# First two heads in pieces, over two queues, in an attention and gated-layer kernel

## The reference, cut to what matters

```python
# 4 batches x 8 heads, 576 positions, head size 64, all float32
scores = scale * np.matmul(q, k.transpose(0, 1, 3, 2))
thresh = np.max(scores, axis=-1, keepdims=True) - tau
scores = np.where(scores >= thresh, scores, -1000000000.0)
scores = scores - np.max(scores, axis=-1, keepdims=True)
attn = np.exp(scores)
attn = attn / (np.sum(attn, axis=-1, keepdims=True) + 1e-09)
x = np.matmul(attn, v)                     # 4 x 576 x 512 after the heads are joined
u = x + (x^T @ U @ V)^T                    # mixing over positions, rank 32
y = u + np.maximum(u @ w_ch1, 0.0) @ w_ch2
out = (sigmoid(causal 5-tap convolution of y) * (y @ w_val)) @ w_out
```

## Time and profile before

| | us |
|---|---|
| median of 3 runs | 836.61 (835.25 to 836.88) |
| profiled execution | 835.42 |
| its span | 833.6 |
| PE busy | 812.9 (98% of the span) |
| DVE busy | 443.4 (53%) |
| ACT busy | 397.4 (48%) |
| POOL busy | 396.6 (48%) |

### The profile page before, as it was taken

How to read it: one execution, slowest core, us unless ns; L and a number is a source line. 1 busy time by engine, 2 the same in 40 slices (tenths; PEclk the granted TensorE clock), 3 DMA queues, 4 the chain that set the end, 5 groups by cost and what they waited for, 6 DMA issues and landing times. The chain is left out here.

```text
span 833.6 us, 17430 instructions
## 1 busy us (share of the span) xinstructions
PE 812.9 (98%) x6864; PEld 770.5 (92%) x6864; DVE 443.4 (53%) x996; ACT 397.4 (48%) x1019; POOL 396.6 (48%) x290
## 2 busy tenths in 40 slices
PE   4999999999999989999999999999999999999998
PEld 4889888899889879999999999999999999988986
DVE  6999999999999854332231322313223123384231
ACT  5999999999999933222121221212212112244231
POOL 4999887788860000082280731905509147191000
PEclk9999999999999999999999999999999999999999
DMA  7444334333422022100000000000000102122221
GB/s 180 115 128 115 85 110 125 104 85 93 125 64 69 2 64 89 39 1 29 1 29 2 1 29 1 2 29 1 29 2 1 54 25 82 37 104 94 80 79 63
DMA packets 27759, 49.36 MB, mean 59 GB/s; under 512 B 5344, under 2 KB 14112, under 8 KB 27680
## 3 DMA queue, kind: packets, MB, share of 16 engines
q1 hardware_dynamic: 24944, 43.54, 18.5%
q10 hardware_dynamic: 2736, 4.72, 1.5%
HBM read 38.81 MB, written 8.85 MB: 57 GB/s over the span
## 5 line engine op out<-in xcount | busy, mean ns | idle before, releaser
L862 DVE SCALAR_TENSOR_TENSOR h_lo<-psum,h_hi 128x288 fp32r<-128x288 f32 x128 | 58.6, 458 | 244.7 <-ACT h_hi L787 244.7
L787 ACT ACTIVATE h_hi<-psum 128x288 fp32r<-128x288 f32 x128 | 52.7, 412 | 256.0 <-PE psum L723 256.0
L721 PE MATMUL psum<-u_split,w_hi 128*128 128x288 f32 x512 | 152.0, 297 | 3.1 <-PEq L135 3.1
L723 PE MATMUL psum<-u_split,w_lo 128*128 128x288 f32 x512 | 152.3, 297 | 0.0
L722 PE MATMUL psum<-u_split,w_hi 128*128 128x288 f32 x512 | 151.8, 297 | 0.0
L494 DVE TENSOR_REDUCE neg_max<-psum 128x1 f32<-128x576 f32 (+1 forms) x160 | 119.2, 745 | 20.4 <-PE psum L254 20.1
L503 DVE SCALAR_TENSOR_TENSOR probs<-psum,thresh,exp_scores 128x576 f32<-128x576 f32 (+1 forms) x160 | 129.3, 808 | 0.8 <-ACT exp_scores L369 0.8
L932 POOL TENSOR_TENSOR conv<-x_t,cw 128x576 f32<-128x576 f32 x14 | 16.1, 1153 | 232.5 <-DVE x_t L870 231.9
L369 ACT ACTIVATE exp_scores<-psum,neg_max 128x576 f32<-128x576 f32 (+1 forms) x160 | 118.1, 738 | 0.0
L253 PE MATMUL psum<-qk_split 128*128 128x288 f32 (+1 forms) x320 | 105.8, 345 | 10.5 <-DVE qk_split L482 9.6
L721 PEld LDWEIGHTS psum<-u_split,w_hi 128*128 128x128 f32 x512 | 97.1, 190 | 3.9 <-issue 3.3
(11 more groups left out here) (127 smaller groups left out, 1900.4 us busy)
## 6 DMA issues: line engine op xcount, KB each, us to landing
qk_raw<-in_qk SPq DMA_DIRECT2D x60, 288.0 KB, 4.3
out<-o_sb ACTq DMA_DIRECT2D x18, 256.0 KB, 2.0
w_stage<-in_w SPq DMA_DIRECT2D x16, 256.0 KB, 3.1
v_main<-in_v SPq DMA_DIRECT2D x16, 256.0 KB, 2.6
conv<-in_w SPq DMA_DIRECT2D x16, 256.0 KB, 2.6
conv_dram<-conv SPq DMA_DIRECT2D x7, 576.0 KB, 2.9
gates<-conv_dram SPq DMA_DIRECT2D x7, 576.0 KB, 3.7
probs<-in_qk SPq DMA_DIRECT2D x4, 288.0 KB, 5.0
```

The costliest lines, as they stand in the source:

```text
L721: nc.tensor.matmul(out, w1_hi[:, cols], u_hi[:, half, d], start=(d == 0), stop=False)
L723: mm = nc.tensor.matmul(out, w1_lo[:, cols], u_hi[:, half, d], start=False, stop=(d == DB - 1))
```

## The change

The four transfers of the first pair become ten, ordered by first use: keys of head 0, the first 128 queries of both heads, keys of head 1, queries 128 to 255, queries 256 to 575. Of the first two pieces the upper partition half is issued by ACT and the lower by SP; all others by SP. They are staged at the end of the tensor `pt`, not in `probs`. ACT applies the scale as it rounds the queries, a piece of both heads at a time; DVE applies it again as it subtracts, in one operation. The order on DVE is: tau's operations, low keys 0, low queries (first piece), low keys 1, maximum(0), low queries (second piece), then the loop. The last piece is rounded by ACT after exponent(0); POOL multiplies it by the scale and subtracts, ahead of its work on the second pair. SP loads the values of the first pair ahead of the first w1 weights. PE waits for the pieces one by one.

```diff
+    QUERIES = [slice(0, P), slice(P, 2 * P), slice(2 * P, S)]
+    pt_flat = pt[:].rearrange("p a b c -> p (a b c)")
+    scaled = pt_flat[:, 0:2 * (S - 2 * P)].rearrange("p (a s) -> p a s", a=2)
+    first_qk = pt_flat[:, 3 * P * (2 * KM + 2) - 4 * S:3 * P * (2 * KM + 2)].rearrange("p (a b s) -> p a b s", a=2, b=2)
+    first_q, first_k = first_qk[:, :, 0], first_qk[:, :, 1]
...
+    def load_first_keys(engine, a, h):
+        engine.dma_start(first_k[D * h:D * h + D, a], qk[a, :, 1]).then_inc(first_k_in[a], 16)
+
+    def load_first_queries(engine, piece, h):
+        engine.dma_start(first_q[D * h:D * h + D, :, QUERIES[piece]],
+                         qk[0:2, :, 0, QUERIES[piece]].rearrange("a d s -> d a s")).then_inc(first_q_in[piece], 16)
...
 # SP
-            for a in range(2):
+            load_first_keys(sp, 0, 0)
+            load_first_queries(sp, 0, 0)
+            for h in range(2):
+                load_first_keys(sp, 1, h)
+            for piece in (1, 2):
                 for h in range(2):
-                    sp.dma_start(probs[D * h:D * h + D, a].rearrange("p (a b) -> p a b", a=2),
-                                 qk[a]).then_inc(first_in[a], 16)
+                    load_first_queries(sp, piece, h)
             for a in range(2):
                 for h in range(2):
                     sp.dma_start(raw[D * h:D * h + D, a], qk[2 + a]).then_inc(qk_in[a], 16)
+            sp.wait_ge(zero_ready, 1)
+            load(0)
             load_w1(0)
-            sp.wait_ge(zero_ready, 1)
-            for p in range(PAIRS):
+            for p in range(1, PAIRS):
                 load(p)
...
 # POOL, ahead of work(1)
+            pool.wait_ge(first_q_in[2], 32)
+            nc.gpsimd.tensor_tensor(scaled[D:P], first_q[D:P, :, QUERIES[2]],
+                                    q_scale[D:P].unsqueeze(2).broadcast_to([D, 2, S - 2 * P]), ALU.mult
+                                    ).then_inc(rest_scaled, 1)
+            pool.wait_ge(rest_scaled, 1)
+            pool.wait_ge(first_q_hi, 3)
+            low = split[D:P, 0:2, 0, QUERIES[2]]
+            nc.gpsimd.tensor_tensor(low, scaled[D:P], low.bitcast(F32), ALU.subtract).then_inc(first_q_split[2], 1)
+            pool.wait_ge(first_q_split[2], 1)
...
 # PE
-                if b == 0 and pair == 0:
-                    pe.wait_ge(first_split, a + 1)
+                if pair == 0 and a == 0 and b < 3:
+                    pe.wait_ge(first_q_split[b], 1)
+                if pair == 0 and b == 0:
+                    pe.wait_ge(first_k_split, a + 1)
...
 # ACT
+            def first_keys_high(a):
+                act.wait_ge(first_k_in[a], 32)
+                nc.scalar.copy(split[:, a, 1], first_k[:, a]).then_inc(first_k_hi, 1)
+
+            def first_queries_high(piece):
+                act.wait_ge(first_q_in[piece], 32)
+                nc.scalar.activation(split[:, 0:2, 0, QUERIES[piece]], first_q[:, :, QUERIES[piece]], ACT.Identity,
+                                     scale=q_scale[:]).then_inc(first_q_hi, 1)
+
+            load_first_keys(act, 0, 1)
+            load_first_queries(act, 0, 1)
             act.wait_ge(one_ready, 1)
             nc.scalar.activation(warm[:], one[:], ACT.Exp)
-            for hd in range(2):
-                act.wait_ge(first_in[hd], 32)
-                nc.scalar.copy(split[:, hd, 1], probs[:, hd, S:2 * S]).then_inc(first_hi, 1)
-                act.wait_ge(q_scaled, hd + 1)
-                nc.scalar.copy(split[:, hd, 0], probs[:, hd, 0:S]).then_inc(first_hi, 1)
             act.wait_ge(tau_ready, 4)
+            first_keys_high(0)
+            first_queries_high(0)
+            first_keys_high(1)
+            first_queries_high(1)
 
             for i in range(STEPS):
                 if i > 1:
                     spread_inverse(i - 2)
                 threshold(2 * i)
                 exponent(2 * i)
+                if i == 0:
+                    first_queries_high(2)
...
 # DVE (the loop over hd of lines 475 to 483 goes; tau's operations come first)
+            def first_keys_low(a):
+                dve.wait_ge(first_k_hi, a + 1)
+                nc.vector.tensor_tensor(k_lo[:, a], first_k[:, a], split[:, a, 1].bitcast(F32),
+                                        ALU.subtract).then_inc(first_k_split, 1)
+
+            def first_queries_low(piece):
+
+                low = split[D:P, 0:2, 0, QUERIES[piece]]
+                dve.wait_ge(first_q_hi, piece + 1)
+                nc.vector.scalar_tensor_tensor(out=low, in0=first_q[D:P, :, QUERIES[piece]], scalar=q_scale[D:P],
+                                               in1=low.bitcast(F32), op0=ALU.mult, op1=ALU.subtract
+                                               ).then_inc(first_q_split[piece], 1)
+
+            first_keys_low(0)
+            first_queries_low(0)
+            first_keys_low(1)
...
             maximum(0)
+            first_queries_low(1)
             for i in range(STEPS):
```

More of the change, by code:

```diff
@@ L108, in attention @@
     v_in = [sem(f"v_in{i}") for i in range(3)]
-    first_in = [sem(f"first_in{i}") for i in range(2)]
+    first_k_in = [sem(f"first_k_in{i}") for i in range(2)]
+    first_q_in = [sem(f"first_q_in{i}") for i in range(3)]
+    first_q_hi = sem("first_q_hi"); first_q_split = [sem(f"first_q_split{i}") for i in range(3)]
+    rest_scaled = sem("rest_scaled")
     w1_in = sem("w1_in")
@@ L112, in attention @@
     zero_ready = sem("zero_ready")
-    q_scaled = sem("q_scaled"); first_hi = sem("first_hi"); first_split = sem("first_split"); part_done = sem("part_done"); split_ready = sem("split_ready")
+    first_k_hi = sem("first_k_hi"); first_k_split = sem("first_k_split"); part_done = sem("part_done"); split_ready = sem("split_ready")
     s_ready = sem("s_ready"); max_done = sem("max_done"); exp_done = sem("exp_done")
@@ L472, in _ @@
             dve.wait_ge(tau_ready, 1)
[L475 to L483, removed]
             nc.vector.tensor_scalar(huge[:], tau_sb[:], 0.0, 3.0e38, ALU.is_lt, ALU.mult).then_inc(tau_ready, 1)
```

## The result

The changed kernel takes 838.48 us (median of 10 runs, 837.62 to 840.48), the kernel before 836.48 us (10 runs, 835.25 to 836.92): ratio 1.0029, interval 1.002 to 1.0037. (The ratios in this document are estimated from all the runs, so they differ a little from those of the medians, here 1.0024.) It is slower by 2.0 us where 2.0 us less were forecast, and lies outside the range. Its profiled execution took 838.64 us with a span of 836.8, against 835.42 and 833.6: 3.2 us more. That is more than the medians differ by, as the profiled execution of before was one of its quicker ones. Two executions behind the experiments, one of the kernel before (3341.85 us) and one of e2 (4478.07 us), are left out of the ratios.

What follows compares the result with a forecast made beforehand. TensorE, at 98% of the span, was taken as the bound, its idle time lying in the wait for the first two heads' splitting. Sum −2.0 us, all from an earlier weights(1), other terms free: 834.6 us, range 833.4 to 836.1.

Steps and rivals of the forecast that it cites:

- The start: Kernel's opening up to weights(1): forecast at 12.57 instead of 14.55, 2.0 us gained, first matmul near 6.7.
- the collision: DVE's low part of the second queries waits for POOL's multiply on the last queries: 0.93 us later, bounds 0 to 1.28.
- the 0.26 us for a faster rate of two queues: First transfers: two issuing queues land the first 416 KB 0.26 us earlier, the middle between 229 and 319 KB per us.
- the formula 3.53 + C/229: First pair's transfers: C KB of the queue land at 3.53 + C/229 us, giving first keys at 4.79.
- what that start gains, all later work gains: All work after weights(1): fixed rhythm of PE, DVE and ACT, nothing tied to absolute time, so the 2.0 us stays.
- the POOL part: POOL's splits from the second pair on: 1.1 us later, head 3's slack falls from 5.0 to 2.0 us, no cost.
- my own term, 1.1 us later: POOL's split of heads 2 and 3 starts at 12.3 instead of 11.23, 1.1 us later, at no cost.
- (a): Rival at the start: no collision on DVE, weights(1) at 11.65, 2.9 us gained, 833.7 us; chance 0.24.
- (b): Rival in first transfers: pieces come no sooner where it counts, only 0.9 us gained, 835.7; chance 0.18 shared with (d).
- (c): Rival on TensorE's early clock rise: if it comes late, 0.48 us lost per us; rise at 26 gives 838.2; chance 0.08.
- (d): Rival: POOL starts head 2 over 2 us after 12.3, PE waits in pair 1; chance 0.18 shared with (b).
- 0.05 for slower: Whole kernel: chance 0.05 that the change makes it slower, against 0.64 faster by over 0.2% and 0.31 within 0.2%.

Runs made afterwards that it cites:

- e2: Kernel before, with one POOL operation of the second pair's first head done twice, same output: 838.15 us, ratio 1.0024 to the kernel before.
- e8: Changed kernel, second queries' low part before maximum(0), second and third w1 chunks rounded in steps 11 and 15, all ten pieces on SP's queue: 833.13 us, ratio 0.9965.
- e4: Changed kernel with DVE's low part of the second queries ahead of maximum(0) instead of behind it: 838.36 us, ratio 1.0034 to the kernel before.
- e9: Changed kernel with SP issuing the second w1 chunk ahead of the fourth pair's values instead of behind them: 836.93 us in one execution.
- e3: Changed kernel with low parts of the last 320 queries made by DVE after weights(0) instead of by POOL: 837.48 us, ratio 1.0019 to the kernel before.
- e1: Changed kernel with ACT's rounding of the second w1 chunk moved from step 9 to step 11: 834.83 us, ratio 0.9987 to the kernel before.

## Why the prediction was wrong

**The start: right.** First matmul 6.75 (near 6.7 forecast), the collision at 1.30 us (1.3), weights(1) at 12.41 (12.57), POOL's first operation of the second pair at 12.29 (12.3), no wait for the fifth unit or for head 3. That the start came out so close is in part luck. Of the transfers the sizes were off and cancelled: first keys 4.33 (4.53), first queries 5.63 (5.09), second keys 6.35 (6.34), last queries 8.65 (8.30). No run shows the 0.26 us for a faster rate of two queues. The keys came before 4.79, the time without it, because the formula 3.53 + C/229, which was counted back from later landings, is too late for the first piece: with one queue they landed at 4.30 (e8). ACT's roundings with the scale took 0.51 and 0.82 us where I had 0.41 and 0.73.

**The step that failed** is in the first part: "what that start gains, all later work gains, since PE, DVE and ACT then run in a fixed rhythm and nothing is tied to an absolute time". The second w1 chunk is tied to POOL's time, through SP's queue: split of head 5, raw loads of head 7, values of pair 3, then the chunk. Its landing does not move with the start, and the kernel before needed it in the very moment it came. e4 shows this in the purest form: a further gain at the start, no gain at the end. I had checked the first w1 chunk and the first values ("needed after 18 us"), and none of the later ones.

**The same fault in the POOL part.** That POOL needs 6.4 us for a head and PE 8.9, "so the slack grows from there", is true of the heads and was taken for POOL as a whole. What POOL's lateness costs runs through the transfers that wait for it, and e2 shows the price: 1.56 us for one more operation of 1.5. By my own term, 1.1 us later, this was worth 0.93 us of the 3.27. With the 1.5 us that the lower clock cost behind the pause, which no term of the sum had, it makes the 2.4 us by which the ratio of 1.0029 has the kernel slower.

**The rivals.** (a) was right that the collision hangs on a thread: the changed kernel's profiled execution had it, with POOL's multiply 0.23 us ahead of DVE's instruction; e9's did not, with DVE 0.12 us ahead. (b) was half seen, first queries at 5.63, without effect on weights(1). (c) gave the sign and a price of the right size, for the wrong place: TensorE did lose its higher level, not because the rise failed to come with the start (matmuls over 288 columns took 0.29 us from 16.04 on, 2 to 3.6 us earlier than before), but in the pause that the missing chunk made. The rate of 0.48 us per us at the lower level fits: the low stretch behind the pause, 0.87 of full clock in the 47th us, 0.50 in the next three and 0.92 in the 51st, makes 3.4 us at half clock, so 1.6, and cost 1.5. That (c)'s 838.2 lies near the measured 838.48 is chance. (d) looked at POOL and stopped at the heads. None named the w1 load.

**The chances.** 0.05 for slower was the chance of the one mechanism I had priced. The list of waits, and the earlier trace rows, had a row with 0.2 us for a transfer, one time; I read it as nothing because it cost nothing.

## What to carry to other kernels

A gain at the start of a pipeline is kept only if everything that is consumed later also comes earlier: for each load and each side engine, compare when it lands with when it is first asked for, for every chunk and not the first alone. A wait of 0.1 or 0.2 us on a transfer is a row to look for: here it marked a deadline with no slack, and each microsecond won ahead of it, or lost on the engine that releases the load, turned into waiting. Where the instruction that waits stands in an engine's written order ahead of work that others need, moving it one or two steps down can be worth more than the change itself (here some 3.5 us for one ACT instruction).

## What the runs showed of the hardware that was not expected

The pause has a price beyond its length. In the changed kernel TensorE stood still for 3.45 us, up to 45.55; at 46.7, when it was at work again, its granted clock fell to 0.5 (0.67 is the mean of the stretch from 45 to 50), and matmuls over 288 columns took 0.44 us again:

```profile
47.65 0.61 PE L284 MATMUL psum<-qk_split 128*128 128x288 f32 x1
48.06 0.44 PE L285 MATMUL psum<-k_lo,qk_split 128*128 128x288 f32 x1
```

A pause of 1.8 us in e2 and one of 3.5 us in e9 left the clock alone; those of 2.3 (e3), 3.4 (after) and 4.6 us (e4) did not. So the length of a pause alone does not say whether the clock falls. The stretch behind it in e9, and then in e3:

```profile
45.00:50.00 5.00, 5.00 (x64) 4.53 (x63) 4.67 (x11) 4.75 (x15) 4.77 (x4) 1.00 0.46 121
```

```profile
45.00:50.00 5.00, 4.80 (x37) 4.28 (x38) 2.64 (x7) 3.19 (x11) 4.76 (x4) 0.66 0.48 118
```

The same falls happen at the change of blocks near 300 us, in every profiled execution, and in some near 740 us (e9, and e1, where it cost 1.5 us between the perceptron's end, 2.03 ahead, and the last matmul, 0.5 ahead).

The mean granted clock of every execution is on record, and 3.4 us at half clock lower it by 0.002. In the profiled execution of before, with one such stretch, it is 0.998; in that of the changed kernel, with one behind the pause and two at the change of blocks, 0.994. Of the 56 executions of the kernel before that the experiments were compared with, the 25 at 0.997 or 0.998 took 835.17 to 835.81 us and the 31 at 0.995 or 0.996 took 836.18 to 837.29. So its two groups are those with and without a further low stretch; where that one falls is not seen. All ten executions of the changed kernel are at 0.992 to 0.996, so each had a further one, and the quickest took 837.62, where the quickest of before, 835.25, plus the 0.93 that is left after step 9, plus 1.5, is 837.7. That fits a clock that fell in the pause in all ten, which is worked out and not seen, as only one was profiled.
